# MLP tasks given out by weight: a plan of TensorE work beside attention, per step

## The reference

```python
# attention: 8 heads of 64, q and k and v are (4, 8, 576, 64)
scores = q @ k.T / 8
scores = where(scores >= max(scores) - tau, scores, -1e9)
x = softmax(scores) @ v                     # heads side by side: (4, 576, 512)
# MLP: token mixing of rank 32, then two dense layers
u = x + ((x.T @ U) @ V).T                   # U (576, 32), V (32, 576)
y = u + relu(u @ w_ch1) @ w_ch2             # (512, 2048), (2048, 512)
# experts: 8 experts, one per row, chosen by logits and a sticky local gate
out[row] = p[e] * (relu(y[row] @ w1[e]) @ w2[e])
```

## Time and profile before

| | |
|---|---|
| median of 3 runs | 1145.09 us (1145.08 to 1146.52) |
| profiled execution | 1144.81 us, span 1143.0 us |
| TensorE busy | 1060.0 us, 93% of the span |
| VectorE, ScalarE, GpSimd busy | 521.7, 471.1, 349.9 us |
| mean granted TensorE clock | 0.973 |
| MLP beside attention (steps 36 to 143) | about 100 to 683 us |
| rest of the last batch's MLP | about 683 to 820 us |

### The profile page before, as it was taken

One profiled execution on the slowest core, in us unless ns is written; L12 is line 12 of the kernel. 1 busy time (PEld: TensorE's weight loads), 2 busy tenths in 40 slices (PEclk: granted clock), 3 DMA queues, 4 the chain that ended last, 5 costly groups with the idle time before them and its releaser, 6 DMA issues. The chain is left out here.

```text
span 1143.0 us, 19941 instructions
## 1 busy us (share of the span) xinstructions
PE 1060.0 (93%) x7054; PEld 922.7 (81%) x7055; DVE 521.7 (46%) x1008; ACT 471.1 (41%) x894; POOL 349.9 (31%) x332
## 2 busy tenths in 40 slices
PE   6998999999789999979999998999759999999995
PEld 5765889999579999957999986999647887787784
DVE  4665544544354454434444542222385533245631
ACT  5775534444454444355444433111233533334630
POOL 4455122543303354330434431452120111111121
PEclk9999999999999999999999998999859999999998
DMA  7886051624335262442415212120256443155511
GB/s 160 192 184 179 19 135 48 162 72 122 123 70 115 68 162 73 124 128 63 114 49 141 74 38 79 47 87 15 96 188 247 144 148 115 58 180 180 180 38 34
DMA packets 110649, 127.26 MB, mean 111 GB/s; under 512 B 67213, under 2 KB 67213, under 8 KB 110544
## 3 DMA queue, kind: packets, MB, share of 16 engines
q1 hardware_dynamic: 104480, 114.54, 35.3%
q0 software_dynamic: 3520, 10.75, 2.9%
q10 hardware_dynamic: 2544, 0.59, 0.2%
HBM read 87.90 MB, written 10.22 MB: 86 GB/s over the span
## 5 line engine op out<-in xcount | busy, mean ns | idle before, releaser
L783 ACT ACTIVATE ex<-score_banks,stat 128x576 f32<-128x576 f32 x132 | 97.9, 741 | 183.0 <-DVE stat L920 183.0
L473 POOL CAST w_hi<-stage 128x1024 fp32r<-128x1024 f32 x64 | 66.6, 1041 | 305.8 <-PE mlp_banks L682 260.4
L682 PE MATMUL mlp_banks<-u_hi,w_hi 128*128 128x320 f32 (+1 forms) x512 | 157.0, 307 | 3.1 <-ACT u_hi L833 2.3
L690 PE MATMUL mlp_banks<-hid_hi,w_hi 128*128 128x320 f32 (+1 forms) x512 | 158.1, 309 | 0.8 <-DVE hid_lo L969 0.8
L929 DVE SCALAR_TENSOR_TENSOR ex<-score_banks,stat,ex 128x576 f32<-128x576 f32 x132 | 107.7, 816 | 108.7 <-ACT stat L787 107.1
L478 POOL TENSOR_TENSOR w_lo<-stage,w_hi 128x1024 fp32r<-128x1024 f32 (+1 forms) x70 | 154.1, 2204 | 4.8
L682 PE MATMUL mlp_banks<-u_hi,w_lo 128*128 128x320 f32 (+1 forms) x512 | 151.4, 296 | 0.0
L690 PE MATMUL mlp_banks<-hid_hi,w_lo 128*128 128x320 f32 (+1 forms) x512 | 151.3, 296 | 0.0
L682 PE MATMUL mlp_banks<-u_lo,w_hi 128*128 128x320 f32 (+1 forms) x512 | 151.3, 296 | 0.0
L690 PE MATMUL mlp_banks<-hid_lo,w_hi 128*128 128x320 f32 (+1 forms) x512 | 151.3, 295 | 0.0
L920 DVE TENSOR_REDUCE stat<-score_banks 128x1 f32<-128x576 f32 x132 | 99.4, 753 | 35.8 <-PE score_banks L615 26.9
(11 more groups left out here) (233 smaller groups left out, 1975.0 us busy)
## 6 DMA issues: line engine op xcount, KB each, us to landing
stage<-in_moe_w_ch SPq DMA_DIRECT2D x64, 512.0 KB, 3.6
w_raw<-in_moe_w SPq DMA_DIRECT2D x64, 512.0 KB, 5.5
q_tiles<-q_parts SPq DMA_DIRECT2D x30, 320.0 KB, 4.4
q_tiles<-q_parts SPq DMA_DIRECT2D x60, 160.0 KB, 4.3
k_tiles<-k_parts SPq DMA_DIRECT2D x60, 144.0 KB, 3.5
raw_q<-in_q SPq DMA_DIRECT2D x32, 128.0 KB, 3.2
raw_v<-in_v SPq DMA_DIRECT2D x32, 128.0 KB, 2.7
raw_k<-in_k SPq DMA_DIRECT2D x28, 128.0 KB, 2.7
```

The lines of the kernel that those rows point to most:

```text
L473: nc.gpsimd.tensor_copy(w_hi[:, n % RING], stage[:, n % 2]).then_inc(w_upper, 1)
L682: last = nc.tensor.matmul(bank[:, 0:w], ch1(a, g, d, c), of[:, d, cols], start=(d == 0 and n == 0), stop=(d == KC - 1 and n == 2))
L690: last = nc.tensor.matmul(bank[:, 0:w], ch2(a, g, q, c), of[:, q, 0:w], start=(q == 0 and n == 0), stop=(q == QUARTER - 1 and n == 2))
L783: nc.scalar.activation(ex_of(n), score_of(n), ACT.Exp, bias=stat[:, n % 4, 0:1], scale=-1.0).then_inc(exp_done, 1)
```

## The change

Only `tasks_by_step` changes. Each kind of task gets a weight, columns times products on TensorE, and each of the nine steps of a pair a weight of its attention work. For a batch the sum of both over the steps is divided into equal shares, and each step takes tasks until half of the next one would go beyond the share. At the start of a batch, the last tasks of the one before are given out in the first two steps; two tasks (`LATE`) are held back for them.

```diff
--- before.py
+++ after.py
@@ -64,6 +64,7 @@
 TASKS = mlp_tasks()
 NTASK = len(TASKS)
 TAIL = 4 + NT
+LATE = 2
 BY_ACT = [k in ("token_mix", "mixed", "hidden", "gate", "rows") for k, *_ in TASKS]
 BY_DVE = [k in ("token_mix", "mixed", "hidden", "channel", "logits") for k, *_ in TASKS]
 GROUP0 = 1 + 2 * KC
@@ -76,29 +77,38 @@
     return sum(by) * batch + sum(by[:m + 1])
 
 
+WEIGHT = {"token_mix": 10240, "mixed": 2048, "hidden": 3 * KC, "channel": 3 * QUARTER, "gate": 512, "logits": 512, "rows": 1024}
+ATTENTION = [11000, 4300, 3200, 2700, 9000, 3200, 2700, 4000, 2700]
+
+
+def weight(t):
+
+    kind, k, *_ = TASKS[t % NTASK]
+    return WEIGHT[kind] * (WIDTH[k] if kind in ("hidden", "channel") else 1)
+
+
 def tasks_by_step():
 
     plan = []
     done = 0
     for n in range(NBLK):
         b, at = divmod(n, ALONE)
-        j = at % STEPS
         if b == 0:
             plan.append([])
             continue
-        ready = NTASK * b - (TAIL if at < ALONE else 0)
-        if b == 1 and at < 2:
-            want = at
-        elif at < 2:
-            ready = NTASK * (b - 1)
-            want = 4 if at == 0 else TAIL
-        elif at == 2:
-            want = 1
+        first = 2 if b > 1 else 1
+        if at < first:
+            take = 0 if b == 1 else LATE + 1 if at == 0 else NTASK * (b - 1) - done
         else:
-            want = 3 if j in (6, 8) else 2
-        if n == NBLK - 1 or at == ALONE - 1:
-            want = PER_GROUP
-        take = max(0, min(want, ready - done))
+            end = NTASK * b - TAIL - (LATE if b < B - 1 else 0)
+            if at == first:
+                rest = sum(weight(t) for t in range(done, end)) + sum(ATTENTION[i % STEPS] for i in range(first, ALONE))
+                share, used = rest / (ALONE - first), 0
+            used += ATTENTION[at % STEPS]
+            take = 0
+            while done + take < end and (at == ALONE - 1 or used + weight(done + take) / 2 < share * (at - first + 1)):
+                used += weight(done + take)
+                take += 1
         plan.append(list(range(done, done + take)))
         done += take
     while done < NTASK * B:
```

## The result

The changed kernel takes 1162.57 us, median of 4 runs (1158.39 to 1163.64), against 1145.8 us (1145.08 to 1146.52) beside it: a ratio of 1.0134, 95% interval 1.0106 to 1.0161. It is slower by 16.8 us; the forecast was 1162. In a later group of runs it was 1161.64, ratio 1.0145 (1.0122 to 1.0168).

The account below looks back on a forecast made before the run. TensorE, busy 1060.0 of 1143.0 us, was taken to bound the kernel. The terms 22.8 - 5.1 - 2.0 + 1.6 = +17.3 us on 1144.8 gave 1162 us, range 1151 to 1170.

Parts of the forecast that it names:

- The saturated stretches: Attention stretches with hidden and channel tasks, TensorE idle 0.00 of 140 us; no order of tasks wins anything there.
- The thin steps: Steps with one task or none, nothing behind turn(n) to cover ScalarE's copy; 20 new ones named, +22.8 us.
- The unit price: Cost of one step with nothing behind turn(n), a distance between starts on TensorE: 1.14 us, bounds 0.79 and 1.14.
- The ends: Last steps of batches, 71, 107 and 143, no longer lack cover behind turn(n): 2.83 + 1.14 + 1.14 = 5.1 us gained.
- Mixed tasks: Batch starts, three or four mixed tasks a step instead of two: waits 13.9 us against 16.0, net -2, bounds -6 to +2.
- hid_lo: First channel product waits for the last hidden task's hid_lo in steps 42, 59, 87, 138: +1.6 us, bounds 0 and 2.
- rows: Step 73, eight tasks instead of five: gate_part wait goes, rows tasks start later: 0, from -1 to +2 us.
- weights: Weight pieces are split three steps or more before first use in both plans, so no cost: 0 us.
- B: Rival: the copy is covered after all in steps j = 0 and 4, kernel faster at 1140 us; chance 0.05.
- C: Rival: a thin step costs about half, 0.6 us, as the delay eats later waits: 1152 us; chance 0.10.
- D: Rival: weight pieces come late, one us in each of the 12 groups: 1174 us; chance 0.03.
- A: Rival: the clock falls two to four times more, +3.4 to +6.8 us, so 1165 to 1169; chance 0.14.

Follow-up runs that it names:

- the ends alone: Kernel before, tasks held back from steps 60, 69, 105 and 141 so the last step before each batch boundary has two: 1141.07 us, ratio 0.9951.
- turn first: Changed kernel, plan kept; in steps with one task, turn(n) and its copy go ahead of the task: 1146.75 us, ratio 1.0007 to the kernel before.
- heavy dose: Kernel before, one task moved from step j = 4 to j = 5 in nine pairs, giving nine more thin steps: 1155.05 us, ratio 1.0088.
- floor of two: Changed kernel, each step taking at least two tasks while there are any, token mix excepted: 1142.34 us, ratio 0.9966 to the kernel before.
- light dose: Kernel before, one task moved from step j = 3 to j = 4 in nine pairs, giving nine more thin steps: 1156.67 us, ratio 1.0086.
- the best of these plans: Kernel before with last steps of batches filled, and turn(n) before a lone task in 37, 38, 74 and 110: 1139.58 us, ratio 0.9942.

## Why the prediction was right

**The saturated stretches: right.** Nothing was won in them, in any plan. TensorE's busy time is 6.7 us higher than before, where the prediction said that it would hardly change. Its own price held this part: only 0.79 us of a thin step are idle, and the rest counts as busy, because nothing overlaps the turn's last transpose and the scores last 0.81 instead of 0.70 us. With the measured price of 1.06 us (below) that is 0.27 us in each of 18 more thin steps, 4.9 us, and one more fall of the clock is 1.7: together 6.6 of the 6.7 us, as an estimate.

**The thin steps: right, in number, place and mechanism.** All 20 named steps have their wait of 0.79 us (0.80 in step 49). The list of waits was misread in the prediction, though: the waits of scores for the copy were 10.4 us and not 7.1, since the entry with step 71 was left out, and they grew by 7.1 us and not by 13, since six waits in the mixed steps changed their cause. The unit price was 1.14 us; it is 1.06. The step that was left out is small and shows in the rows of the changed kernel: the first product of a task is followed after 0.20 us when the task stands behind a turn, and after 0.12 us when it stands behind scores; a thin step has no task behind its turn and saves these 0.08 us.

```profile
340.68 0.28 PE L700 MATMUL mlp_banks<-hid_hi,w_hi 128*128 128x256 f32 x1
340.80 0.28 PE L700 MATMUL mlp_banks<-hid_lo,w_hi 128*128 128x256 f32 x1
...
342.57 0.36 PE L700 MATMUL mlp_banks<-hid_hi,w_hi 128*128 128x256 f32 x1
342.77 0.28 PE L700 MATMUL mlp_banks<-hid_lo,w_hi 128*128 128x256 f32 x1
```

Five of the nine heavy thin steps, where nothing else moved, cost 1.04 to 1.09 us each by the starts of equal steps.

**The ends: right.** -5.1 predicted; with the same 0.08 three times -4.9; the ends alone measured -4.8, and their interval leaves 3.8 to 7.4.

**Mixed tasks: right sign, size off, within its bounds.** Forecast -2.0. The three stretches were idle for 4.0, 4.3 and 4.2 us before; now, to the same task of their batch or a little further:

```profile
110.19:138.34 28.15, 23.59 (x187) 21.48 (x188) 13.61 (x31) 14.77 (x37) 3.35 (x3) 1.00 0.11 38
315.60:349.80 34.20, 30.85 (x237) 29.25 (x238) 16.38 (x37) 17.17 (x44) 4.29 (x4) 0.95 0.42 104
519.13:554.30 35.17, 31.12 (x236) 28.41 (x237) 16.46 (x37) 17.27 (x44) 4.28 (x4) 0.95 0.43 101
```

4.6, 3.4 and 4.1 us idle: about -0.5 visible and some -1.2 with the 0.25 us a wait that doesn't show, an estimate. The wait for the third task was 1.42 us where 1.5 was worked out, that at step 77 1.89 and that at step 113 1.40 where it was 2.0.

**hid_lo, rows, weights.** Waits for hid_lo: 0.16 to 0.29 us visible in steps 42, 59, 87 and 138, 0.78 in all and about +1.2 with what doesn't show (an estimate), where +1.6 was forecast. Steps 72 and 73: the wait for gate_part is gone, and gates (0.97), z_rows (0.24) and z_rows (1.58) cost 2.79 us where 0.89 + 1.00 + 0.89 = 2.78 were; 0 was right. No wait for a weight piece appears.

**The sum.** 21.2 - 4.9 - 1.2 + 1.2 + 1.7 (one more fall of the clock) = +18.0 us at step 144, where the first product starts at 683.42 before and at 701.56 now: +18.1. The whole execution is 17.2 longer. Behind step 144, where both plans are the same, 1 us comes back: at 711 us of the kernel before the distance is 17.73, and behind one wait near the end of the experts, 5.30 us instead of 5.82, it is 17.09. Why these waits are shorter stays open.

That +17.3 met this so closely is luck. The unit price that was too dear (1.6 us over 20 steps) nearly made up for a fall of the clock that the sum left out (1.7); the gain at the mixed tasks was put 0.8 us too large, and 1 us came back behind step 144. The mechanism, the steps and the size of its main term don't hang on this.

**Rivals.** B (the copy is covered) is refuted by turn first and by the heavy dose: long work in front of the turn covers nothing, the same work behind it does. C (half the price) too: 1.06 by the starts, and 0.75 to 1.5 by the times of the heavy dose, not 0.6. D (weight pieces come late): no such wait. A (the clock) is real but small. In the changed kernel's profile there was one fall more, not two to four, and what it does can be read from single executions: 1158.04 us at a mean clock of 0.979 and 1166.59 at 0.973; in the kernel without attention weights 1141.76 at 0.978 and 1148.99 at 0.972; in the kernel before 1142.64 at 0.979 and 1152.06 at 0.970. This spread is of every plan here. Nothing shows that the changed plan makes falls more frequent: its mean granted clock over 6 executions is that of the kernel before (0.9738).

## What to carry to other kernels

When two engines hand a bank back and forth in a fixed order, count what stands behind the instruction that is waited for, not the work of the step: 1.5 us of products behind the transpose hid the whole copy here, 2.3 us in front of it hid none. A plan that balances load gained nothing where the bounding engine had no idle time, and lost wherever it left a step without that cover; a lower limit of two tasks was worth 20 us here, and issuing the transpose before a lone task 16. Look at the ends of each phase first: three badly filled steps held 4.8 of the 5.8 us that the best of these plans gained.

## What the runs showed of the hardware

Beside attention, the granted clock fell to its lower level, 1.2 GHz, for 3.4 us at a time. In the profiles TensorE had waited shortly before each fall, several times in a row (0.79 and 1.84 us before the one at 115 us; 1.42 and 1.89 before the one at 330) or once for 2.48 (floor of two, 283 us; light dose, 294 us). It didn't fall at each such place: the kernel before has the same 2.48 us at 290 us without a fall. The executions of one kernel differ by 4 to 10 us, 0.4 to 0.9%, and their mean granted clocks lie between 0.969 and 0.979, the slower ones mostly lower. Apart from the changed kernel and the two doses, the plans differ by less than that, so one execution of each doesn't rank them.

What a product costs depends on what it follows: the next start comes 0.20 us after the first 256-column product behind a transpose and 0.12 us after one behind the scores, and four products of 288 columns take 0.54 us after a task and 0.64 us after a wait or after values.
